# Weight slices and the first x tile loaded and split earlier in a delta-rule scan, four value quads asked for ahead of it, and each inverse stored first in its step

## The reference

```python
for t in range(S):                                   # 768 tokens, 32 heads of 48
    kt, vt, bt = (k_n[:, :, t], v[:, :, t], beta[:, :, t, None])
    y[:, :, t] = np.einsum('bhd,bhde->bhe', q[:, :, t], state)
    v_old = np.einsum('bhde,bhd->bhe', state, kt)
    state = state + bt[:, :, :, None] * np.einsum('bhd,bhe->bhde', kt, vt - v_old)
# x: 3072 tokens x 384
h = x @ w_in                                         # 384 x 2048
g = (a0 + a1*h + a2*h^2 + a3*h^3) / (1 + |b0|*|h| + |b1|*h^2 + 1e-6)
x = g @ w_out                                        # 2048 x 384
out = max(x @ w2_in, 0)**2 @ w2_out
```

## Time and profile before

| | |
|---|---|
| median of 3 runs | 1115.49 us (1114.19 to 1116.07) |
| profiled execution | 1117.83 us, span 1116.1 us |
| granted TensorE clock, mean | 0.994 |
| PE busy | 1093.1 us (98%) |
| DVE, ACT, POOL busy | 672.9, 650.7, 499.9 us |
| DMA | 74.42 MB, mean 67 GB/s |

### The profile page before, as it was taken

How to read it: one execution, slowest core, us unless ns; L and a number is a source line. 1 busy time by engine, 2 the same in 40 slices (tenths; PEclk the granted TensorE clock), 3 DMA queues, 4 the chain that set the end, 5 groups by cost and what they waited for, 6 DMA issues and landing times.

```text
span 1116.1 us, 18346 instructions
## 1 busy us (share of the span) xinstructions
PE 1093.1 (98%) x6370; PEld 943.6 (85%) x6370; DVE 672.9 (60%) x1087; ACT 650.7 (58%) x1277; POOL 499.9 (45%) x807
## 2 busy tenths in 40 slices
PE   8799999999999999999999999999999999999998
PEld 6599999999987888888888888888888888888887
DVE  6976555433559978788887889854343433334332
ACT  5576666544669878777877778653333333333322
POOL 5284887683029977787887778500000000000000
PEclk9999999999999999999999999999999999999999
DMA  9847887556432110010101003140100101010000
GB/s 210 180 99 165 162 168 160 122 98 165 107 96 82 43 57 1 13 44 1 57 1 57 1 7 102 49 128 1 57 1 0 58 1 56 1 57 1 1 29 29
DMA packets 174043, 74.42 MB, mean 67 GB/s; under 512 B 136000, under 2 KB 161728, under 8 KB 172992
## 3 DMA queue, kind: packets, MB, share of 16 engines
q1 hardware_dynamic: 164352, 68.54, 25.4%
q10 hardware_dynamic: 9600, 4.72, 1.7%
HBM read 52.27 MB, written 20.71 MB: 65 GB/s over the span
## 4 chain that ended last, share of the span: by engine, by line
PE 91%; DVE 4%; issue 2%; DMA 1%; SPq 1%; POOL 1%; ACT 1%; ACTq 0%; POOLq 0%; DVEq 0%
PE ps L1174 12%; PE ps L1176 12%; PE ps L1175 12%; PE ps L1162 11%; PE ps L1160 11%; PE ps L1161 11%; PE ps L542 3%; PE ps L519 3%; PE ps L572 3%; PE ps L586 3%; PE ps L552 3%; PE ps L558 3%; PE ps L589 2%; PE ps L502 1%; PE ps L600 1%
## 5 line engine op out<-in xcount | busy, mean ns | idle before, releaser
L1160 PE MATMUL ps<-x_split,weights 128*128 128x512 f32 x576 | 225.1, 391 | 3.2 <-DVE g_lo L1319 2.3
L1162 PE MATMUL ps<-x_split,weights 128*128 128x512 f32 x576 | 224.8, 390 | 0.0
L1161 PE MATMUL ps<-x_split,weights 128*128 128x512 f32 x576 | 224.6, 390 | 0.0
L1174 PE MATMUL ps<-g_hi,weights 128*128 128x512 f32 x576 | 224.4, 390 | 0.1
L1175 PE MATMUL ps<-g_lo,weights 128*128 128x512 f32 x576 | 224.1, 389 | 0.0
L1176 PE MATMUL ps<-g_hi,weights 128*128 128x512 f32 x576 | 224.1, 389 | 0.0
L1329 DVE TENSOR_TENSOR common<-common 128x512 f32<-128x512 f32 x96 | 66.3, 691 | 135.0 <-ACT common L1233 133.4
L1239 ACT ACTIVATE g_hi<-common 128x512 fp32r<-128x512 f32 x96 | 60.7, 633 | 141.9 <-PE ps L1176 137.4
L1160 PEld LDWEIGHTS ps<-x_split,weights 128*128 128x128 f32 x576 | 108.4, 188 | 26.1 <-DVE g_lo L1319 2.8
L1378 POOL TENSOR_SCALAR common<-common,b_abs 128x512 f32<-128x512 f32 x96 | 74.7, 778 | 121.3 <-ACT common L1208 121.3
L1392 POOL TENSOR_TENSOR common<-common,g_hi 128x512 f32<-128x512 f32 x96 | 124.7, 1299 | 9.4 <-DVE g_hi L1307 9.4
(11 more groups left out here) (118 smaller groups left out, 1904.1 us busy)
## 6 DMA issues: line engine op xcount, KB each, us to landing
scan_late<-kq_in SPq DMA_DIRECT2D x10, 768.0 KB, 6.0
scan_late<-kq_in SPq DMA_DIRECT2D x16, 384.0 KB, 4.3
shared<-w_in SPq DMA_DIRECT2D x32, 192.0 KB, 2.4
shared<-w_out SPq DMA_DIRECT2D x32, 192.0 KB, 2.6
x_first<-y_t ACTq DMA_DIRECT2D x24, 192.0 KB, 2.9
shared<-x_first SPq DMA_DIRECT2D x6, 768.0 KB, 5.8
x_second<-shared SPq DMA_DIRECT2D x6, 768.0 KB, 4.2
shared<-x_second SPq DMA_DIRECT2D x6, 768.0 KB, 5.8
```

Of the source, the lines that this page charges most:

```text
L1160: pe.matmul(bank(n), lo, x_hi[:, slot, k, :], start=(k == 0), stop=False)
L1161: pe.matmul(bank(n), hi, x_lo[:, slot, k, :], start=False, stop=False)
L1162: mm = pe.matmul(bank(n), hi, x_hi[:, slot, k, :], start=False, stop=(k == KT - 1))
L1174: pe.matmul(ps_y[m], lo, g_hi[:, d, :], start=(f == 0), stop=False)
```

## The change

There are four edits.

1. `W_LOADS` says in which SP step each weight slice is loaded: slices 0 and 1 in 31 and 32, 2 and 3 in 35 and 36, 4 and 5 in 37, 6 and 7 in 39, 8 to 13 in 42 to 47. Slices 0 and 1 take slots 0 and 1, slices 2 and 3 take the same slots again, and slices 4 and 5 take slots 2 and 3 first (`raw_slot`, `raw_former`). x is loaded in step 33.
2. `W_SPLITS` puts the splits into steps 33, 34, 36, 37 and 41 to 46 (`PRE` = 10), `X_SPLITS` those of x into 38, 39 and 40. Steps 47 and 48 have none.
3. `load_v` of quads 2 to 7 is issued before step 0; it was quad 2 before it, and quads 3 to 7 in steps 2, 6, 10, 14, 18.
4. `store_inverse` is the first in its step, ahead of `load_cross`, `load_kq` and `store_n`. That changes the order in steps 6 and 13.

```diff
-    FF_LOADS, FF_SPLIT, FF_X = GROUPS - 11, GROUPS - 8, (41, 43, 45)
+    W_LOADS = {31: (0,), 32: (1,), 35: (2,), 36: (3,), 37: (4, 5), 39: (6, 7), 42: (8,), 43: (9,), 44: (10,), 45: (11,),
+               46: (12,), 47: (13,)}
+    W_SPLITS = {33: 0, 34: 1, 36: 2, 37: 3, 41: 4, 42: 5, 43: 6, 44: 7, 45: 8, 46: 9}
+    X_LOAD, X_SPLITS = 33, (38, 39, 40)
...
-            load_v(2)
+            for h in range(2, RING // 4):
+                load_v(h)
             for n in range(LAST_MM):
+                for r in range(1, ROUNDS):
+                    if n == INV_OUT[r]:
+                        store_inverse(r)
...
-                for r in range(1, ROUNDS):
-                    if n == INV_OUT[r]:
-                        store_inverse(r)
...
-                for h in range(3, QUADS):
+                for h in range(RING // 4, QUADS):
                     if n == 4 * h - 10:
                         load_v(h)
-                if n == FF_LOADS:
+                if n == min(W_LOADS):
                     ff.load_ab(sp)
-                    ff.load_weights(sp, 0)
+                for i in W_LOADS.get(n, ()):
+                    ff.load_weights(sp, i)
+                if n == X_LOAD:
                     ff.load_x(sp, 0)
-                    for i in range(1, ff.W_SLOTS):
-                        ff.load_weights(sp, i)
-                if 0 <= n - FF_LOADS - 2 < ff.PRE:
-                    ff.load_weights(sp, n - FF_LOADS - 2 + ff.W_SLOTS)
...
-                if 0 <= n - FF_SPLIT < ff.PRE:
-                    ff.split_weights_hi(act, n - FF_SPLIT)
+                if n in W_SPLITS:
+                    ff.split_weights_hi(act, W_SPLITS[n])
...
-    W_SLOTS, W_AHEAD, PRE = 4, 3, 9
+    W_SLOTS, W_AHEAD, PRE = 4, 3, 10
...
+    def raw_slot(i):
+        return i if i < 2 else (i + 2) % W_SLOTS
+
+    def raw_former(i):
+        return {2: 0, 3: 1}.get(i, i - W_SLOTS if i >= 6 else None)
...
-        if i >= W_SLOTS:
-            sp.wait_ge(w_lo_ready, i - W_SLOTS + 1)
+        if raw_former(i) is not None:
+            sp.wait_ge(w_lo_ready, raw_former(i) + 1)
```

More of the change, by code:

```diff
@@ L773, in _ @@
                     take_z_first(n)
-                if n in FF_X:
-                    ff.split_x_hi(act, FF_X.index(n), 0)
+                if n in X_SPLITS:
+                    ff.split_x_hi(act, X_SPLITS.index(n), 0)
                 spread = (n + 1 + LEAD) // 2 if n > TWICE[1] and n % 2 == 1 and end_group(n + 1) is not None else None
@@ L999, in _ @@
                         scale_v(h)
-                if n == FF_SPLIT:
+                if n == min(W_SPLITS):
                     ff.coef_bounds(dve)
[L1002 to L1005, removed]
+                if n in W_SPLITS:
+                    ff.split_weights_lo(dve, W_SPLITS[n])
+                if n in X_SPLITS:
+                    ff.split_x_lo(dve, X_SPLITS.index(n), 0)
             ff.vector(dve, ys_done, GROUPS)
@@ L1088, in bank, with raw_loads @@
         return ps_h[n % H_BANKS]
+    def raw_slot(i):
+        return i if i < 2 else (i + 2) % W_SLOTS
+    def raw_former(i):
+        return {2: 0, 3: 1}.get(i, i - W_SLOTS if i >= 6 else None)
+    def raw_loads(i):
+        return 1 if i < 2 else (i + 2) // W_SLOTS + (raw_slot(i) < 2)
     def load_ab(sp):
@@ L1095, in load_weights @@
     def load_weights(sp, i):
-        m, f, slot = i // FT, i % FT, i % W_SLOTS
-        if i >= W_SLOTS:
-            sp.wait_ge(w_lo_ready, i - W_SLOTS + 1)
+        m, f, slot = i // FT, i % FT, raw_slot(i)
+        if raw_former(i) is not None:
+            sp.wait_ge(w_lo_ready, raw_former(i) + 1)
         sp.dma_start(w_raw[:, slot, 0:D_MODEL].rearrange("p (k n) -> p k n", k=KT),
@@ L1192, in split_weights_hi @@
         f = i % FT
-        act.wait_ge(w_loaded[i % W_SLOTS], 32 * (i // W_SLOTS) + 32)
+        act.wait_ge(w_loaded[raw_slot(i)], 32 * raw_loads(i))
         if i >= FT:
@@ L1196, in split_weights_hi @@
             act.wait_ge(down_done, UNITS - FT + f + 1)
-        act.activation(weights[:, f, 0:2 * D_MODEL], w_raw[:, i % W_SLOTS], ACT.Copy).then_inc(w_hi_ready, 1)
+        act.activation(weights[:, f, 0:2 * D_MODEL], w_raw[:, raw_slot(i)], ACT.Copy).then_inc(w_hi_ready, 1)
     def split_x_hi(act, k, tile):
@@ L1283, in split_weights_lo @@
         dve.wait_ge(w_hi_ready, i + 1)
-        dve.tensor_tensor(weights[:, f, 2 * D_MODEL:4 * D_MODEL], w_raw[:, i % W_SLOTS],
+        dve.tensor_tensor(weights[:, f, 2 * D_MODEL:4 * D_MODEL], w_raw[:, raw_slot(i)],
                           weights[:, f, 0:2 * D_MODEL].bitcast(F32), ALU.subtract).then_inc(w_lo_ready, 1)
```

## The result

The changed kernel takes 1118.44 us (median of 12 runs, 1115.66 to 1120.03) where the one before, run beside it, takes 1115.51 (12 runs). The ratio is 1.0022, with a 95% interval of 1.0011 to 1.0032: slower, by about the least that can be told. The forecast was 1111.9. It was wrong in its sign, and the time lies outside the range.

A forecast was written before the change was run, and what follows sets the result against it. PE was taken as the bound (91% of the chain), with only its stalls in the first 345 us counting. Terms -3.8 + 3.9 + 1.2 - 1.3 - 3.6 = -3.6 us gave 1114.2, less 2.34: 1111.9 us, range 1107.6 to 1114.6.

The forecast's parts named there:

- step 9: In the scan, the wait for quad 8's keys ends: -2.13 of idle, -1.7 of half clock, -3.8 us.
- step 7: In the scan, quad 7's keys come 2.2 us later behind the inverse store, and the clock falls: +3.9 us.
- step 37: In the scan, PE's cross part waits for slice 2's split, clock staying up: +1.2 us, bounds 0.1 and 3.4.
- step 44: In the scan, PE's wait of 1.28 us for quad 11's inverses goes, their loads leaving earlier: -1.3 us.
- unit 6: At the network's start, PE's idle of 2.33 us shrinks by 1.9 and the clock's fall (1.7) goes: -3.6 us.
- Slices 2 and 3, step 36: SP issues these loads behind round 5's inverse store and quad 11's values; slice 2 lands at 267.2: +1.2 us.
- rival C: The wait for slice 2 makes the clock fall: +3.4 + 1.7 instead of +1.2, 1115.8 us; chance 0.10.
- rival D: Early loads of values fill the queues, quad 6's keys come 5.6 us late, clock falls: 1119.2 us; chance 0.06.
- the clock behind unit 6: At the network's start, the fall of the clock over 4.4 us no longer happens: -1.7 us.
- the values ahead of the scan: Four added issues before step 0 fit SP's idle stretch, done 7 us before quad 6's keys: no cost.
- rival A: Quad 7's keys aren't held up by the inverse store: +0.4 in place of +3.9, 1108.4 us; chance 0.27.
- B: The network's filling keeps its clock fall, or step 9's wait is only shortened: -1.9, 1113.6 us; chance 0.15.

The follow-up runs named there:

- before_again: The kernel before, unchanged, run once more for a second profile: 1116.0 us, ratio 0.9995.
- h_sbuf: The kernel before with four added DVE instructions of 128x512 in steps 28, 29, 30 and 32, both inputs in SBUF: 1119.31 us, one run.
- e_best: The changed kernel with inverse stores back in their old place, slices 2 and 3 ahead of round 5's store, quad 7's keys issued in step 5: 1108.52 us.
- e_w_first: The changed kernel with weight slices 2 and 3 issued ahead of round 5's inverse store and quad 11's values: 1114.09 us, ratio 0.9965.
- e_v_behind: The changed kernel with slices 2 and 3 issued right behind round 5's inverse store but ahead of quad 11's values: 1113.95 us, ratio 0.9985.
- e_net_only: The kernel before with only the new loads and splits of weights and x, plus slices 2 and 3 ahead of round 5's inverse store: 1112.91 us.
- e_values: The kernel before with only the values of quads 3 to 7 also loaded ahead of the scan: 1113.91 us, ratio 0.9969.
- e_inv_only: The kernel before with only the store of the inverses moved first in its step: 1117.79 us, ratio 1.0016.
- h_psum: The kernel before with four added DVE instructions of 128x512 in steps 28, 29, 30 and 32, one input in PSUM: 1117.14 us, one run.
- e_both: The changed kernel with inverse stores back in their old place and slices 2 and 3 ahead of round 5's store: 1109.95 us, ratio 0.9933.

## Why the prediction was wrong

By the two profiles, each term as forecast and as measured:

| | forecast | measured | |
|---|---|---|---|
| step 9 | -3.8 | -4.0 | idle gone, clock 1.00 |
| step 7 | +3.9 | +3.15 | idle +1.84, clock +1.3 |
| **step 37** | **+1.2** | **+4.9** | **idle 3.14, clock 1.7** |
| step 44 | -1.3 | -1.5 | |
| unit 6 | -3.6 | -2.6 | idle -1.7, from unit 6 to the end -0.9 |
| start of the scan | 0 | +0.6 | |
| sum | -3.6 | +0.5 | |

The clock's part of a row is what the starts of PE's matmuls leave beside the idle; for step 7 that is 1.3, where window times lost clock gives 1.7. The start of the scan differs from one execution to the next: it is 0.4 later than in the first profile in `before_again` and 1.4 in `h_sbuf`, which have nothing changed there, and 0.1 in `e_best`, which has the early values. So the 0.6 isn't put down to the change.

**The step that failed is "Slices 2 and 3, step 36".** The place and the order of events were right: store, values, slice, split, z. The size was not, in three ways. It let the store leave at 261.07, as before. It left at 262.92, since the splits that this change moves into steps 33 and 34 hold up POOL's inversion; the prediction had those splits at nothing because DVE and ACT have idle time there, and didn't ask who else would feel them. It let the first DMA of slice 2 take its usual half microsecond; with the store and the values in the queue the issue took 2.11. The values' own issue was 1.0 shorter than forecast (0.43 for 1.43), so the second DMA of slice 2 left 2.4 late, at 265.94, and what was left of its way took 3.1 where the forecast had 3.7. That puts the landing at 269.04, 1.8 late, near the upper bound of 269.4 and not shortly behind 266.5. And the idle of 3.14 was then long enough for the clock to fall, for 1.7 more. That is rival C, given 0.10; its total of +5.1 for this place against 4.9 measured is near. (Its total of 1115.8 isn't, for the reason under "The base"; that rival D's 1119.2 is the nearest number is luck, since nothing of D happened.) Its evidence "for" should have weighed more than the choice of a value shortly behind the values. `e_w_first` shows that the place decides it, and `e_v_behind` that the values in between are most of it.

The rule that was missed stands in the Trainium skill ("SBUF — State Buffer", "Who interferes with whom"): a DVE instruction with two SBUF inputs contends with a GpSimd instruction that reads SBUF, and the port pair that they share is an exclusive lock. The trace agrees, with 0.60 to 0.72 us a time. The kernel before had shown it too, in one POOL instruction of 1.35 us (128x240, at 241.41) under DVE's `scale_v` of 241.34, with 0.61 for its neighbour of the same shape.

**A second term was mis-sized: the clock behind unit 6.** The prediction took 4.4 x 0.39 = 1.7 us for it. From unit 6 to the end it is 774.5 us before and 773.5 now, 0.9 less. And `h_sbuf`, which has the start of the network as before, had the stall without the fall:

```profile
343.25 0.50 PE L1164 MATMUL ps<-x_split,weights 128*128 128x512 f32 x1 [2.34 <-DVE g_lo L1323]
...
368.56 0.50 PE L1164 MATMUL ps<-x_split,weights 128*128 128x512 f32 x1 [0.27 <-DVE g_lo L1323]
...
373.20 0.50 PE L1164 MATMUL ps<-x_split,weights 128*128 128x512 f32 x1 [0.27 <-DVE g_lo L1323]
```

```profile
343.20:347.60 4.40, 4.35 (x19) 3.58 (x20) 4.38 (x7) 4.37 (x8) 4.32 (x5) 1.00 0.02 4
```

Its matmuls were 1.55 us ahead of those of before 20 matmuls behind unit 6, and had only 0.15 of it left at the end (774.35 for 774.47 from unit 6 on): at full clock PE comes to the later units sooner and waits for g_lo, as the two 0.27 show. DVE, ACT and POOL are busy for nearly all of these 4.4 us, which fits that they set the pace there; which of them does isn't shown. In the kernel before, that fall cost 0.1 to 0.2 us and not 1.7. The changed kernel is 1.6 ahead at the same point and keeps 0.95; 0.26 of what it gives back is the wait for g_lo at 372.22. `e_net_only` has the same 773.5, so it is the new plan of loads and splits that gives the 0.9. One execution without the fall is few, but the four others with the stall and the fall (`before_again`, `e_values`, `e_inv_only`, `h_psum`) end within 0.1 us of 774.5.

**Right:** the values ahead of the scan. Four issues took 7.14 us, 1.8 each, and ended 7 us ahead of the keys of quad 6 (73.38), so rival D fell. The term of step 9 holds in `e_values` with 3.5 us of the median. The store before the keys: ACT got them 2.5 us later than before, of which 0.7 is the later start of the scan; its wait grew by 1.83 and PE's idle by 1.84, a little under the 2.2 taken and well over the 0.4 of rival A, which this excludes. Step 44 holds: its first load leaves at 287.85, where 283.5 was estimated for a scan that is then 4.7 us further on. Unit 6 holds in its stall (0.99) and in the clock of 1.00 behind it, which excludes B; what that clock was worth is told above.

**The base.** Even with step 37 right, the median would have come out too low. The forecast carried the 2.34 by which the profiled execution of before stands above its median over to the changed kernel. The changed kernel's profile (1118.34) stands at its median (1118.44). By the profiles the change costs 0.5 us, by the medians 2.9, and nearly all of the difference is this. A fall of the clock isn't a fixed price. Behind about the same stall it cost 1.7 in one execution and 3.0 in another (step 7, 2.87 and 3.06 of idle), nothing in four more (2.58 in `e_v_behind`, 2.55 in `e_net_only`, 2.38 in step 9 of `h_psum`, 2.34 ahead of unit 6 in `h_sbuf`), and 1.7 by the window behind a mere 2.13 and 2.17 in the two profiles of before. Up to step 28 `h_psum` is the kernel before, so that kernel's fall in step 9 is there in some of its executions and not in others. Over all the profiles of this case, a fall followed each of the seven stalls of 2.87 to 3.35 us, and eight of the twelve of 2.13 to 2.58. The changed kernel's stalls (2.87 to 3.14) are of the first kind, those of before (2.13 to 2.40) of the second. That would put the median of before under its two profiles, which both had both falls, and leave the changed kernel's where its profile is, as measured. But it is a count over different steps and kernels, and the fall at unit 6 costs next to nothing, so the 2.34 stay open.

`e_both` is the changed kernel without the two costs of order: 1109.95 on a chip where before takes 1117.59.

## What to carry to other kernels

An issue's place in a DMA queue's program isn't its place in time: a wait far ahead of it, for another engine, holds it back, so loads whose slots are long free belong in front of such a wait, and what an engine waits for in front of bulk stores and loads. Moving DVE work with two SBUF inputs to a place where "DVE is idle" isn't free while GpSimd works on something that others wait for. And a fall of TensorE's clock seen in one profile is a price with a spread: take it at its full size in no more than one case of a forecast, look at a second profile before subtracting it, and ask whether PE waits for other engines soon behind it, since then most of it can be given back.

## What the runs showed of the hardware

- DVE and POOL exclude each other where DVE reads two inputs from SBUF: 0.60 to 0.72 us for POOL under a DVE instruction of 128x768 in the changed kernel (0.74 in the one before), 0.3 to 0.5 under one of 128x512, none with an input in PSUM. DVE's own instruction is lengthened in turn (0.93 for 0.68, 1.14 for 0.95).
- A store of 512 KB issued 0.5 us ahead of 768 KB of loads in the same queue landed 3.3 us after its issue, and the loads 7.4 after theirs. The other way round it was 5.9 for the loads and 8.2 for the store.
- An issue of 192 KB took SP 2.11 us behind the store and 384 KB of values in rows of 192 bytes; straight behind the store it took 0.43, and the next one 0.87.
- The clock's fall after a stall of 2.1 to 3.4 us took anything from 0 to 3.0 us by the window. Behind unit 6 of the network, where ACT, DVE and POOL are busy throughout, full clock instead of the fall was worth 0.1 to 0.2 us.
